# The recurrent attention's gates are prepared for the first 128 positions alone, the rest between steps, and the split of the weights' low halves is spread over more steps

## The reference

```python
for t in range(S):                                  # S = 768, B = 4, H = 8, D = 40
    m_new = np.maximum(f_gate[:, :, t] + m, i_gate[:, :, t])
    f_stab = np.exp(f_gate[:, :, t] + m - m_new)
    i_stab = np.exp(i_gate[:, :, t] - m_new)
    m = m_new
    C = f_stab[:, :, None, None] * C + i_stab[:, :, None, None] * np.einsum('bhd,bhe->bhde', vt, kt)
    n = f_stab[:, :, None] * n + i_stab[:, :, None] * kt
    h_tilde = np.einsum('bhde,bhe->bhd', C, qt)
    nq = np.einsum('bhd,bhd->bh', n, qt)[:, :, None]
    y[:, :, t] = h_tilde / np.maximum(np.abs(nq), 1.0) / (1.0 + np.exp(-o_gate[:, :, t]))
# x = y as (3072, 320): each row goes through relu(x @ w1[e]) @ w2[e] of its best expert e (F = 1024),
# times its gate; then h = x @ w_in, max(0.01 h, h) @ w_out (inner width 2048)
```

## Time and profile before

| | before |
|---|---|
| median of 3 runs | 889.83 us (886.2 to 891.64) |
| profiled execution | 890.42 us, its span 888.7 us |
| TensorE busy | 765.5 us, 86% of the span |
| VectorE busy | 553.8 us, 62% |
| ScalarE busy | 389.6 us, 44% |
| GpSimd busy | 151.1 us, 17% |
| read from and written to memory | 74.85 MB and 23.89 MB |

### The profile page before, as it was taken

One profiled execution on the slowest core, in us unless ns is written; L12 is line 12 of the kernel. 1 busy time (PEld: TensorE's weight loads), 2 busy tenths in 40 slices (PEclk: granted clock), 3 DMA queues, 4 the chain that ended last, 5 costly groups with the idle time before them and its releaser, 6 DMA issues.

```text
span 888.7 us, 17741 instructions
## 1 busy us (share of the span) xinstructions
PE 765.5 (86%) x6459; PEld 560.0 (63%) x6460; DVE 553.8 (62%) x1430; ACT 389.6 (44%) x706; POOL 151.1 (17%) x198
## 2 busy tenths in 40 slices
PE   0879888888637789999999989999999899999994
PEld 0668777777526668888887855555555455555552
DVE  7668987779685755676467755545555355454441
ACT  2345535556353547556455323343343333433432
POOL 4224343444321111111110000010010100100101
PEclk9989999899868999999999999999999999999997
DMA  4798699883015697478740000000000000000000
GB/s 115 205 253 220 199 326 286 241 262 94 24 30 163 238 301 256 142 273 277 251 138 7 2 1 1 1 31 1 1 31 1 31 0 0 30 0 0 30 1 30
DMA packets 49214, 99.79 MB, mean 112 GB/s; under 512 B 7630, under 2 KB 38030, under 8 KB 46574
## 3 DMA queue, kind: packets, MB, share of 16 engines
q1 hardware_dynamic: 40030, 67.72, 25.2%
q10 hardware_dynamic: 6464, 22.02, 7.2%
q0 software_dynamic: 2640, 9.01, 3.0%
HBM read 74.85 MB, written 23.89 MB: 111 GB/s over the span
## 4 chain that ended last, share of the span: by engine, by line
PE 61%; DVE 16%; DMA 7%; issue 7%; ACT 4%; SPq 3%; POOL 1%; DVEq 0%; ACTq 0%; POOLq 0%
PE bank L1424 25%; PE bank L1559 13%; PE bank L1458 11%; PE bank L1304 2%; DMA d_x<-slot 2%; DVE slot L920 2%; PE bank L1329 2%; DMA d_x<-og 2%; ACT stage L793 2%; DVE qk L1244 2%; DVE sxt L1219 1%; PE bank L1414 1%; ACT stage L810 1%; DVE stage L1239 1%; DMA vv<-v_in 1%
## 5 line engine op out<-in xcount | busy, mean ns | idle before, releaser
L1424 PE MATMUL bank<-stage,slot 128*128 128x512 f16 x768 | 181.3, 379 | 0.0
L1559 PE MATMUL bank<-slot,dec 128*128 128x320 f16 x768 | 160.5, 301 | 18.1 <-DVE qk L1244 13.2
L1239 DVE TENSOR_TENSOR stage<-bank,stage 128x512 f32<-128x512 f32 x96 | 66.4, 692 | 108.9 <-ACT stage L793 105.0
L1424 PE MATMUL bank<-qbd,slot 128*128 128x128 f16 x1984 | 117.8, 221 | 13.4 <-issue 13.4
L1424 PEld LDWEIGHTS bank<-qbd,slot 128*128 128x128 f16 x1984 | 113.7, 99 | 16.7 <-issue 16.4
L1424 PEld LDWEIGHTS bank<-stage,slot 128*128 128x128 f16 x768 | 75.2, 98 | 74.1
L1559 PEld LDWEIGHTS bank<-slot,dec 128*128 128x128 f16 x768 | 73.3, 98 | 69.8 <-DVE qk L1244 23.8
L1559 PE MATMUL bank<-slot,qk 128*128 128x320 f16 x384 | 115.3, 300 | 0.0
L793 ACT ACTIVATE stage<-bank 128x512 f32<-128x512 f32 x96 | 57.4, 598 | 130.4 <-PE bank L1424 130.4
L1458 PE MATMUL bank<-slot,emov 128*128 128x320 f16 x496 | 103.2, 302 | 3.4 <-issue 2.2
L1244 DVE TENSOR_TENSOR qk<-stage,dec 128x512 f16<-128x512 f32 x96 | 66.3, 691 | 52.0 <-ACT dec L797 52.0
(11 more groups left out here) (256 smaller groups left out, 1172.5 us busy)
## 6 DMA issues: line engine op xcount, KB each, us to landing
slot<-d_w SPq DMA_DIRECT2D x12, 1280.0 KB, 5.7
d_w<-slot ACTq DMA_DIRECT2D x4, 2560.0 KB, 10.2
stage<-wB SPq DMA_DIRECT2D x6, 1280.0 KB, 8.6
stage<-wA SPq DMA_DIRECT2D x6, 1024.0 KB, 6.0
d_w<-slot SPq DMA_DIRECT2D x4, 1280.0 KB, 9.8
stage<-wB ACTq DMA_DIRECT2D x4, 1280.0 KB, 12.7
qk<-qkT SPq DMA_DIRECT2D x12, 360.0 KB
slot<-qkT SPq DMA_DIRECT2D x12, 360.0 KB
```

Source lines behind the costliest of these rows:

```text
L1239: v.tensor_tensor(fgl[f % 2], bank[f % 2][:, :], ft[f % 2], ALU.max).then_inc(f_g, 1)
L1424: ins = t_.matmul(pf, a[:, col:col + P], x(k), start=(q == 0), stop=(q == len(ops) - 1))
L1559: ins = t_.matmul(bank[4 + q][:, 0:DM], x[f % 2][:, q * P:(q + 1) * P], slotB[2 + f // NF][:, c0:c0 + DM], start=(f == 0 and z == 0), stop ...
```

## The change

The gate chain is cut. Before the first step VectorE handles positions 0 to 127 alone (sums, maximum, the split into parts, now stored by ScalarE's queue in one DMA), then the sums and maxima of the other five chunks. The split of the other 640 positions stands behind the VectorE work of step 0 (first half) and step 1 (second half). ScalarE takes the ten other exponentials at the end of step 0, TensorE transposes them at the end of step 1, and SP stores the rest of the parts and loads the decays (`rest_of_gates`, `decays`) in `reload(2)`. The gates' work area moves from the weight slots to `xreg`. GpSimd clears all four sets of buffers (sets 2 and 3 in `late_set`, before and after its first `keys`), ScalarE clears six other tiles; VectorE clears only `esta` of sets 0 and 1, ahead of the chain. bf16 fills are written as 32-bit words, half as many elements. SP loads the inputs of steps 0 and 1 at once, each kind as its buffer is clear, then unit 2's weights, then the inputs of steps 2 and 3.

In chunk 0 the product with the state is left out, `combine` is one copy and `advance` one multiplication. The tables are new: 15 steps (6 to 20) have one `low` each, nearly always at place 2, where before 8 steps had two each and 4 had one.

```diff
             for b in range(2):
-                load(0, b)
+                load_k(0, b)
+                load_o(0, b)
+                sp.wait_ge(set_done, SETS[b])
+                load_q(0, b)
                 load_v(0, b)
-                load_o(0, b)
-            sp.wait_ge(wl_copied, 1)
-            sp.dma_start(d_wl, gnl[:, :]).then_inc(wl_stored, 16)
-            sp.wait_ge(gate_chain, GATE_PARTS)
-            sp.dma_start(d_negm.rearrange("n r s -> r n s"), gparts[:, 0:3, :]).then_inc(parts_stored, 16)
-            sp.dma_start(d_b.rearrange("n r s -> r n s"), gparts[:, 3:6, :]).then_inc(parts_stored, 16)
-            sp.wait_ge(parts_stored, 32)
-            sp.wait_ge(gate_chain, GATE_ALL)
-            for b in range(2):
-                load_e(0, b)
-
-            sp.wait_ge(wl_stored, 16)
-            for j in range(GH):
-                n = sum(heads(g) > j for g in range(NG))
-                for b in range(B):
-                    src = d_wl[b * H + j:b * H + j + GH * (n - 1) + 1:GH, :]
-                    sp.dma_start(wlr[j * D:(j + 1) * D, b * NG:b * NG + n, :],
-                                 src.partition_broadcast(D)).then_inc(wl_landed, 16)
             load_A(2)
             load_B(2)
+            sp.wait_ge(act_const, 6)
+            for g in range(NG):
+                r = heads(g) * D
+                sp.dma_start(wgt[0:r, g, 0:NE], wg_in[GH * D * g:GH * D * g + r, :]).then_inc(wg_landed, 16)
+            sp.wait_ge(parts_stored, 16)
+            for b in range(2, B):
+                load_k(0, b)
+                load_o(0, b)
+                sp.wait_ge(set_done, SETS[b])
+                load_q(0, b)
+                load_v(0, b)
+                load_e(0, b)
+
+            def rest_of_gates():
+
+                sp.wait_ge(gate_chain, GATE_ALL)
+                sp.dma_start(d_parts[:, :, P:S].rearrange("n r s -> r n s"), gpr).then_inc(rest_stored, 16)
+                sp.wait_ge(wl_copied, 1)
+                sp.dma_start(d_wl, gnl[:, :]).then_inc(wl_stored, 16)
+
+            def decays():
+
+                sp.wait_ge(wl_stored, 16)
+                for j in range(GH):
+                    n = sum(heads(g) > j for g in range(NG))
+                    for b in range(B):
+                        src = d_wl[b * H + j:b * H + j + GH * (n - 1) + 1:GH, :]
+                        sp.dma_start(wlr[j * D:(j + 1) * D, b * NG:b * NG + n, :],
+                                     src.partition_broadcast(D)).then_inc(wl_landed, 16)
...
-                    load(c2, b2)
+                    load_q(c2, b2)
+                    load_k(c2, b2)
                     sp.wait_ge(pv_done, NG * (st - 1))
+                    if st == 2:
+                        rest_of_gates()
+                        sp.wait_ge(rest_stored, 16)
                     load_e(c2, b2)
...
+                if st == 2:
+                    decays()
+                if st in LOAD_A and LOAD_A[st] != 3:
+                    sp.wait_ge(lo_done, lows_until(SPLITS[SPLITS.index(LOAD_A[st]) - 2]))
                 if st in LOAD_A:
-                    sp.wait_ge(lo_done, lows_until(SPLITS[SPLITS.index(LOAD_A[st]) - 2]))
                     load_A(LOAD_A[st])
...
-            sp.wait_ge(rest_done, 2 * REST)
-            for b in range(2, B):
-                load(0, b)
-                load_e(0, b)
-                load_v(0, b)
-                load_o(0, b)
-            load_A(3)
-            load_B(3)
...
+                g.memset(qbd[i][:, :, :], 0.0).then_inc(set_done, 1)
+                g.memset(vv[i][:, :], 1.0).then_inc(set_done, 1)
+                g.memset(emov[i][:, :].bitcast(F32), TWO_ONES).then_inc(set_done, 1)
...
+            def late_set(i):
+
+                g.memset(qbd[i][:, :, :], 0.0).then_inc(set_done, 1)
+                g.memset(vv[i][:, H * D1:VW], 1.0).then_inc(set_done, 1)
+                g.memset(emov[i][:, :].bitcast(F32), TWO_ONES).then_inc(set_done, 1)
+                g.memset(esta[i][:, :].bitcast(F32), 0.0).then_inc(set_done, 1)
+                pool.wait_ge(set_done, SETS[i] - 1)
+                g.memset(esta[i][0:3, :].bitcast(F32), TWO_ONES).then_inc(set_done, 1)
...
+            for i in range(2):
+                fill(num[i][:, :, :].rearrange("p h d -> p (h d)"), one, H * (D1 + 1))
+            fill(xT[:, 2, :], zero, P)
+            fill(xw[:, 3 * P:], zero, 3 * PVN)
+            fill(wlr[:, :, :].rearrange("p b c -> p (b c)"), zero, B * NG * NC)
+            fill(state[:, :, :, :].rearrange("p b g d -> p (b g d)"), zero, B * NG * GH * D1)
+
+            def stable(c):
                 cs = slice(c * P, (c + 1) * P)
                 a.activation(gW[:, cs], gM[:, cs], ACT.Exp, bias=gm0[:, c:c + 1], scale=-1.0).then_inc(gate_exp, 1)
                 a.activation(gG[:, cs], gb[:, cs], ACT.Exp, bias=gnl[:, c:c + 1]).then_inc(gate_exp, 1)
-            act.wait_ge(gate_exp, 2 * NC)
-            act.copy(gnl[:, :], gW[:, P - 1::P]).then_inc(wl_copied, 1)
+
+            act.wait_ge(gate_chain, GATE_FIRST)
+            stable(0)
+            act.wait_ge(gate_chain, GATE_PARTS)
+            act.dma_start(d_parts[:, :, 0:P].rearrange("n r s -> r n s"), gp0).then_inc(parts_stored, 16)
             act.wait_ge(gate_tr, 1)
-            act.copy(wgc[:, :, :, :].rearrange("p c k r -> p (c k r)"), psT[:, 0:NC * 2 * BH]).then_inc(wgc_done, 1)
+            act.copy(wgc[:, 0, :, :].rearrange("p k r -> p (k r)"), psT[:, 0:2 * BH]).then_inc(wgc_done, 1)
+            act.wait_ge(set_done, SETS[1])
+            act.wait_ge(parts_stored, 16)
+            for b in range(2):
+                act.dma_start(emov[b][0:3, :].rearrange("r (h t) -> r h t", h=H),
+                              d_parts[0:3, b * H:(b + 1) * H, 0:P]).then_inc(in_landed[b], 16)
+                act.dma_start(esta[b][3:6, :].rearrange("r (h t) -> r h t", h=H),
+                              d_parts[3:6, b * H:(b + 1) * H, 0:P]).then_inc(in_landed[b], 16)
+
+            def stable_rest():
+
+                act.wait_ge(gate_chain, GATE_SCAN)
+                for c in range(1, NC):
+                    stable(c)
+                act.wait_ge(gate_exp, 2 * NC)
+                act.copy(gnl[:, :], gW[:, P - 1::P]).then_inc(wl_copied, 1)
+
+            def weights_rest():
+
+                act.wait_ge(gate_tr, 2)
...
+            for i in range(2):
+                link(v.memset(esta[i][:, :].bitcast(F32), 0.0))
+                link(v.memset(esta[i][0:3, :].bitcast(F32), TWO_ONES))
+
+            def running(c):
                 cs = slice(c * P, (c + 1) * P)
                 link(v.tensor_tensor_scan(gM[:, cs], gr0[:, cs], gb[:, cs], gm0[:, c:c + 1], ALU.mult, ALU.max))
                 link(v.tensor_tensor(gm0[:, c + 1:c + 2], gM[:, (c + 1) * P - 1:(c + 1) * P],
                                      gF[:, (c + 1) * P - 1:(c + 1) * P], ALU.add))
-            link(v.tensor_scalar(gnl[:, :], gM[:, P - 1::P], -1.0, None, ALU.mult))
+
+            def parts(to, src, sign, lo, hi):
+                link(v.tensor_scalar(to[:, 0, :], src[:, lo:hi], sign, None, ALU.mult))
+                link(v.scalar_tensor_tensor(gr0[:, lo:hi], src[:, lo:hi], sign, to[:, 0, :], ALU.mult, ALU.subtract))
+                link(v.tensor_copy(to[:, 1, :], gr0[:, lo:hi]))
+                link(v.tensor_tensor(to[:, 2, :], gr0[:, lo:hi], to[:, 1, :], ALU.subtract))
+
+            dve.wait_ge(gates_landed, 32)
+            link(v.tensor_tensor_scan(gF[:, 0:P], gr0[:, 0:P], gf[:, 0:P], 0.0, ALU.mult, ALU.add))
+            link(v.tensor_tensor(gb[:, 0:P], gi[:, 0:P], gF[:, 0:P], ALU.subtract))
+            running(0)
+            link(v.tensor_scalar(gnl[:, 0:1], gM[:, P - 1:P], -1.0, None, ALU.mult))
+            assert n[0] == GATE_FIRST, n[0]
+            parts(gp0[:, 0:3, :], gM, -1.0, 0, P)
+            parts(gp0[:, 3:6, :], gb, 1.0, 0, P)
+            assert n[0] == GATE_PARTS, n[0]
+            for c in range(1, NC):
+                cs = slice(c * P, (c + 1) * P)
+                link(v.tensor_tensor_scan(gF[:, cs], gr0[:, cs], gf[:, cs], 0.0, ALU.mult, ALU.add))
+            link(v.tensor_tensor(gb[:, P:S], gi[:, P:S], gF[:, P:S], ALU.subtract))
+            for c in range(1, NC):
+                running(c)
+            link(v.tensor_scalar(gnl[:, 1:NC], gM[:, 2 * P - 1::P], -1.0, None, ALU.mult))
...
+                if c == 0:
+                    v.tensor_copy(num[j][:, GH * g:GH * g + nh, 0:D1],
+                                  psO[i][:, 0:nh * PVN].rearrange("p (h d) -> p h d", h=nh)[:, :, 0:D1]).then_inc(comb_done, 1)
+                    return
                 w = wgc[:, ds(c, 1), 0, b * H + GH * g:b * H + GH * g + nh].rearrange("p c h -> p (c h)")
                 v.tensor_tensor(num[j][:, GH * g:GH * g + nh, 0:D1], psO[i][:, INT:INT + nh * D1].rearrange("p (h d) -> p h d", h=nh),
...
+                if c == 0:
+                    v.tensor_tensor(state[0:r, b, g, 0:w], psU[0:r, 0:w], bdm[0:r, 0:w], ALU.mult).then_inc(st_mid, 1)
+                    return
...
```

(42 more changed lines are left out.)

171 lines of the change are left out of this document (72 added, 99 removed), and 18 rows, old and new, of tables (HIGHS, LOWS, SQUARES).

## The result

The changed kernel takes **855.07 us** (median of 4 runs, 853.72 to 860.35) against 888.47 for the one before: ratio 0.963, 95% interval 0.958 to 0.969. The forecast was 863, range 846 to 880. The sum was made for a profiled execution, and that came at 860.35 (span 858.6) against the forecast's 863.4. It is the slowest of the four, 5.3 us above their median, at the lowest granted TensorE clock (mean 0.969; the others have 0.973 to 0.981). The total is right.

| part | forecast | measured in the two profiled executions |
|---|---|---|
| start to D(0) | 40.9 to 27.9, -13.0 | to 37.42, **-3.5** |
| D(0) to D(5) | -0.8 | **-4.4** (42.5 to 38.2) |
| D(5) to D(20) | -13.2 | **-16.8** (129.2 to 112.4) |
| D(20) to D(23) | 0 | **-0.6** (22.2 to 21.6) |
| behind D(23) | 0 | **-4.9** (653.9 to 649.0) |

What follows compares the result with a forecast made beforehand. TensorE was taken to bound a step at about 6.9 us, DMA close behind. From 890.4 profiled, 13.8 up to D(5) and 13.2 for steps 6 to 20 gave 863.4, as a median 863 us; range 846 to 880.

Steps and rivals of the forecast that it cites:

- D(0): D(n) is the time of step n's denominator row, one a step; step 0's was forecast at 27.9 us against 40.88.
- D(5): Time of the denominator row of attention step 5: forecast 69.6 us against 83.40 before, 13.8 earlier.
- rival D: Start: the small store waits behind the loads, first matmul at 21, 7 us more, 870 in all; chance 0.04.
- I take 14, and 13 to 21 as ends: Start: first matmul of a step at 14 us; 21 if the small store waits for 4.8 MB of loads.
- they share the DMA engines with that round trip: Start: inputs of steps 0 and 1 (2.0 MB) beside the parts' store and load back; 13.3 taken as 14.
- The SP queue's stall: SP's store wait, decay loads and unit 3 delay inputs of steps 5 and 6: 5 us counted, 0 to 11.
- store, decays, unit 3, then step 5: SP's order after the split ends (about 36 us): step 5's inputs arrive near 58, wanted near 54.
- Rival A: Steps 6 to 20: a low costs its time wherever it stands, 8.1 us a step, 879 in all; chance 0.10.
- B: Steps 6 to 14: DMA becomes the bound, each input comes late, 12 us more, 875 in all; chance 0.13.
- C: No DMA waits, loads standing further apart: 11 us less, 852 in all; chance 0.10.
- E: Slower than before: SP's queue never drains, steps 6 to 20 wait for issue, 900 at 9.7 a step; chance 0.03.
- Rival F: Steps 0 to 3: VectorE or ScalarE paces, so omitting the state's product loses 3 us: 866; forecast including it 0.60.

Runs made afterwards that it cites:

- the idle writes: Kernel before the change plus 23 or 64 one-column VectorE writes of a tile nobody reads: 884.40 and 882.66 us, one run each, against 890.87.

## Why the prediction was right or wrong

**The total was right with errors that cancel, and that is luck.** The start fell short by 9.5 us; the steps after D(0) made up 7.8 of that, and what lies behind D(23), which the sum had at 0, 4.9 more.

**Start: a term mis-sized, by the mechanism of rival D.** "I take 14, and 13 to 21 as ends": it was 26.2, beyond my end. The step that failed is "they share the DMA engines with that round trip", priced at 0.7 us. The store took 9.3 us and the load behind it 6.5 up to the matmul; with unit 2 and the inputs of steps 2 and 3 held back the term is 14.8, as forecast. I gave D 0.04 because ScalarE's store has its own queue. That reading went with the rule of the Trainium skill, "DMA: Bandwidth & Descriptors", section "Queues, rings and completion order", by which an engine takes turns between queues packet by packet. The traces do not bear out what I drew from it: the store took 9.3 us with unit 2 ahead, the first 5.0 of them without a packet, and 3.3 with the 2.0 MB of inputs alone; how long a turn is, they do not show. The 21 had priced the store's wait and not the load's that follows it. The terms behind it hid a part: the first `weigh` came 2.4 us behind the matmul (forecast 1.5), but from there D(0) took 8.8 us where I had 12.4 for step 0, the slow start and the split's share, so a matmul 12.2 late made D(0) 9.5 late.

**The split.** 7.7 was forecast, 10.3 measured; 1.5 of it is GpSimd's clearing beside a cast. I had said that the clearing costs VectorE nothing. The Trainium skill's sentence ("SBUF — State Buffer", section "Who interferes with whom"), that an instruction with two SBUF inputs does not contend with one that only writes, says nothing of a cast, which has one input. For the cast the rows show 1.84 and 0.30. The halves of the later split took 2.7 and 3.1 us, as forecast 2.6.

**Steps 1 to 5.** The -0.8 was -4.4. Step 1 took 7.0 (forecast 8.8), steps 2 and 3 6.1 and 6.7 (6.1). The SP queue's stall, priced at 5, showed as 9.1 and 9.3 us for steps 4 and 5, 2.7 more than the 7.0 + 8.7 of their work: after a late start the inputs are less late. TensorE's waits for v of steps 5 and 6 are 1.8 and 1.4, where I had some 5 in all. The experiments show that this is one account: 12 us gained at D(0) leave 4.7 at D(5), as the forecast chain "store, decays, unit 3, then step 5" says. So the start's gain and the queue's price can't be added, as I did.

**Steps 6 to 20.** -13.2 was -16.8, with the mechanism right: 112.4 against 116. Two terms were too dear, the scales (8.28 in place of 8.65, three times) and DMA waits (6, measured about 4: steps 15 and 16 took 9.80 and 7.99, 3.8 above two of 7.0). TensorE's wait itself was only 1.84 of that. Behind it, from 147.4 to 150.6 us, the granted clock was 0.50, the lower of its two levels (1.2 GHz), and a group's scores took 1.58 us against 0.86 in the next step. A DMA wait can so cost about twice its length, but need not: behind the 1.82 us at 63.75 the clock stayed at 1.00. Rival A is refuted at place 2 and would have been true at place 0, 8.0 a step. B did not happen: at a DMA share of 0.98 TensorE was busy 13.97 of 14 us. C, no DMA waits, did not happen either, nor E.

**Rival F held in its outcome and not in its reason.** The product gives 1.85 us by D(3), and 0.1 of it is left at D(10). F put this down to VectorE or ScalarE pacing steps 0 to 3; it is the wait for step 5's inputs that takes it back.

**Behind: 0 was wrong by 4.9.** 3.8 of it is the dense stage, where the kernel before has the wait that the idle writes took away. The other 1.1 lies in the experts' stage, 247.4 to 263.0 us in fourteen profiles with the same code, so it says nothing about the change. TensorE is busy 232 to 238 us of it at a mean granted clock of 0.99 to 0.97, so a part of the spread goes with the clock; what sets the rest is open. Shifting the changed kernel's VectorE program alone gave 250.5 to 251.8 against 254.0.

## What to carry to other kernels

A small store whose landing the first matmul waits for must be issued before the bulk, also when the bulk is in another queue: here its place was worth 11 to 12 us of the start. What is gained at a start is kept only up to the next transfer that the same queue has to make, so add the gain and the queue's price as one chain. And where in a full step a piece of work stands can matter more than how many pieces it holds: the same `low` at place 2 and not at place 0 was worth 15 us.
